# Turning r with VectorE from blocks instead of with TensorE, from the seventh chunk on

## The reference

```python
for t in range(S):
    cur = np.einsum('bhd,bhe->bhde', u[None] * kt, vt)
    y[:, :, t] = np.einsum('bhd,bhde->bhe', rt, state + cur)
    state = wt[:, :, :, None] * state + np.einsum('bhd,bhe->bhde', kt, vt)
...
h = x @ w_in                       # (3072, 384) @ (384, 2048)
g = np.maximum(0.01 * h, h)
x2 = g @ w_out
...
expert_idx = np.argmax(logits, axis=1)      # of the normalised x2 and 8 embeddings
h = np.maximum(x2[mask] @ w1[e], 0.0)
out[mask] = gate_w[mask, None] * (h @ w2[e])
```

## Time and profile before

| what | before |
|---|---|
| median of 3 runs | 835.03 us (833.4 to 835.28) |
| the profiled execution | 834.27 us, its span 832.3 us |
| granted TensorE clock, of full speed | 0.999 |
| TensorE matmuls busy | 814.6 us (98%) |
| VectorE busy | 564.4 us (68%) |
| ScalarE busy | 438.8 us (53%) |
| GpSimd busy | 203.3 us (24%) |

### The profile page before, as it was taken

One profiled execution on the slowest core, in us unless ns is written; L12 is line 12 of the kernel. 1 busy time (PEld: TensorE's weight loads), 2 busy tenths in 40 slices (PEclk: granted clock), 3 DMA queues, 4 the chain that ended last, 5 costly groups with the idle time before them and its releaser, 6 DMA issues.

```text
span 832.3 us, 18049 instructions
## 1 busy us (share of the span) xinstructions
PE 814.6 (98%) x5633; PEld 763.7 (92%) x5633; DVE 564.4 (68%) x1315; ACT 438.8 (53%) x924; POOL 203.3 (24%) x286
## 2 busy tenths in 40 slices
PE   6999999999999999999999999999999999999997
PEld 6899999999999999999999999999889998898896
DVE  6879788879889878879888855635452512545463
ACT  6675564464464465465456435553552533565563
POOL 5611111122103013103113001303343323334433
PEclk9999999999999999999999999999999999999999
DMA  9975432155242141232210001414531513376392
GB/s 215 206 150 130 77 68 39 34 92 69 51 73 34 31 84 33 39 83 38 39 34 30 1 16 30 171 47 128 168 124 40 185 47 100 134 259 201 92 315 66
DMA packets 165307, 78.56 MB, mean 94 GB/s; under 512 B 135486, under 2 KB 153253, under 8 KB 165090
## 3 DMA queue, kind: packets, MB, share of 16 engines
q1 hardware_dynamic: 156402, 64.81, 32.3%
q0 software_dynamic: 4544, 10.85, 4.0%
q10 hardware_dynamic: 4272, 1.82, 0.9%
HBM read 112.90 MB, written 11.63 MB: 150 GB/s over the span
## 4 chain that ended last, share of the span: by engine, by line
PE 85%; SPq 7%; DVE 3%; issue 2%; ACT 1%; DMA 1%; POOL 0%; DVEq 0%; ACTq 0%; POOLq 0%
PE bank L1065 22%; PE bank L1044 21%; PE bank L1117 13%; PE bank L1153 13%; SPq L458 3%; PE bank L1134 3%; PE bank L970 2%; PE bank L937 2%; PE bank L998 2%; PE bank L993 2%; SPq L483 1%; PE bank L1099 1%; PE bank L978 1%; SPq L471 1%; SPq L490 1%
## 5 line engine op out<-in xcount | busy, mean ns | idle before, releaser
L1044 PE MATMUL bank<-xhl,WRh 128*128 128x384 f32 x768 | 219.0, 339 | 0.7 <-DVE WRl L1715 0.5
L1044 PEld LDWEIGHTS bank<-xhl,WRh 128*128 128x128 f32 x768 | 141.3, 188 | 1.2 <-issue 1.2
L1411 ACT COPY gw<-bank 128x384 f32<-128x384 f32 x128 | 61.6, 481 | 152.3 <-PE bank L1044 150.9
L1065 PE MATMUL bank<-WRh,gh 128*128 128x384 f32 x384 | 135.8, 354 | 0.0
L1044 PE MATMUL bank<-xhl,WRl 128*128 128x384 f32 x384 | 130.0, 339 | 0.0
L1065 PE MATMUL bank<-WRh,gl 128*128 128x384 f32 x384 | 129.8, 338 | 0.0
L1065 PE MATMUL bank<-WRl,gh 128*128 128x384 f32 x384 | 129.7, 338 | 0.0
L1734 DVE TENSOR_TENSOR gl<-gw,gh 128x384 fp32r<-128x384 f32 x128 | 72.2, 564 | 56.6 <-ACT gh L1417 52.7
L1417 ACT CAST gh<-gw 128x384 fp32r<-128x384 f32 x128 | 65.2, 510 | 76.7 <-DVE gw L1727 64.4
L1727 DVE SCALAR_TENSOR_TENSOR gw<-gw 128x384 f32<-128x384 f32 x128 | 75.7, 592 | 31.3 <-ACT gw L1411 30.9
L1902 DVE TENSOR_TENSOR hl<-bank,hh 128x512 fp32r<-128x512 f32 x56 | 36.1, 686 | 84.0 <-ACT hh L1452 83.7
(11 more groups left out here) (199 smaller groups left out, 1639.7 us busy)
## 6 DMA issues: line engine op xcount, KB each, us to landing
stage<-in_moe_w_dram SPq DMA_DIRECT2D x96, 768.0 KB
Kn<-in_k_dram SPq DMA_DIRECT2D x24, 192.0 KB, 3.4
Vn<-in_v_dram SPq DMA_DIRECT2D x24, 192.0 KB, 3.2
x_moe<-x2s SPq DMA_DIRECT2D x24, 192.0 KB, 2.0
Rn<-in_r_dram SPq DMA_DIRECT2D x21, 192.0 KB, 2.8
wraw<-in_moe_w_out_dram SPq DMA_DIRECT2D x4, 768.0 KB, 7.4
eraw<-in_moe_w_dram SPq DMA_DIRECT2D x4, 768.0 KB, 8.9
Wn<-in_w_dram SPq DMA_DIRECT2D x152, 16.0 KB, 1.8
```

The source lines that it names most:

```text
L1044: mm = pe.matmul(bank[F_BANK[n % 2]][:, 0:GN], win(t_)[:, f // 4, k_, cols], xhl[G % 2][:, a, k_, :], start=(k_ == 0 and n_ == 0), stop=(k ...
L1065: mm = pe.matmul(bank[O_BANK[i]][:, 0:DM], a[:, z, cols], wout(t_)[:, f, :], start=(f == 0 and n_ == 0), stop=(f == FT - 1 and n_ == 2))
L1411: act.copy(gw[:, n % 2, :], bank[F_BANK[n % 2]][:, 0:GN]).then_inc(s_g0, 1)
```

## The change

From chunk 6 on (`R_BLOCKED = 2 * GT`), r is loaded twice: in its natural form as before, which GpSimd's `products` still need, and in blocks as w is, by 16 DMAs of `load_blocks`, into one of two further places of `Rn` (slot 3, a new one, and slot 2, freed for it). GpSimd clears the padding of these two (`s_pad`). VectorE's new `turn_r` turns the blocks in one instruction, from SBUF right into the bank from which `Rh` is made, at the head of `decay_rk`. TensorE turns only k, into the first of the three banks (`k_bank`) instead of the third. The waits that guarded r's and k's banks (`s_sx`, `s_yhi`, `s_ylo`) stand in front of the scores now. The natural r has two slots from chunk 6 on, so `next_load` waits for a later product. To make room, v has two slots instead of three; v of chunk m + 2 is asked for where v of chunk m + 3 was, and the first v loads move on SP: v of chunk 2 from the very start to where v of chunk 3 was, and so on.

```diff
+        R_BLOCKED = 2 * GT
+        def r_slot(m):
+            return m % NSLOT if m < R_BLOCKED else m % 2
+        def r_blocks(m):
+            return NSLOT - m % 2
+        def k_bank(m):
+            return banks(m)[0 if m >= R_BLOCKED else 2]
...
             def next_load(m):
 
                 sp.wait_ge(s_kT, m - NSLOT + 1)
-                sp.wait_ge(s_rk, m - NSLOT + 1)
+                sp.wait_ge(s_rk, m - NSLOT + 1 if m < R_BLOCKED else m - 1)
...
+            def next_r(m):
+
+                if m < R_BLOCKED + 2:
+                    sp.wait_ge(s_pad, m - R_BLOCKED + 1)
+                else:
+                    sp.wait_ge(s_rT, m - 1)
+                load_blocks(sp, m, r, Rn, r_blocks(m), s_rblk[m % 2])
...
             def next_v(m):
 
-                sp.wait_ge(s_ym, m - NSLOT + 1)
-                sp.wait_ge(s_sm, states(m - NSLOT + 1))
+                sp.wait_ge(s_ym, m - 1)
+                sp.wait_ge(s_sm, states(m - 1))
                 load_v(m)
...
             load_weights(0)
             next_load(GT)
-            next_v(GT)
+            next_v(GT - 1)
             load_weights(1)
...
             next_load(GT + 1)
+            next_v(GT)
             load_weights(2)
             next_v(GT + 1)
             load_weights(3)
             next_load(GT + 2)
-            next_v(GT + 2)
             next_w(GT + 2)
...
+                for m in at(turn_at, n - 2):
+                    if R_BLOCKED <= m + 2 < NC:
+                        next_r(m + 2)
...
                 if m > 2:
                     pe.wait_ge(s_mk, last + 1)
+                if 2 < m < R_BLOCKED:
                     pe.wait_ge(s_sx, states(last + 1))
-                turn_one(m, Rn, banks(m)[1], s_rT)
+                if m < R_BLOCKED:
+                    turn_one(m, Rn, banks(m)[1], s_rT)
...
-                turn_one(m, Kn, banks(m)[2], s_kT)
+                turn_one(m, Kn, k_bank(m), s_kT)
 
             def scores(m):
                 a_, b_, c_ = banks(m)
                 pe.wait_ge(s_rh, m + 1)
                 pe.wait_ge(s_kt, m + 1)
+                if m >= R_BLOCKED:
+                    pe.wait_ge(s_sx, states(m))
+                    pe.wait_ge(s_yhi, m)
+                    pe.wait_ge(s_ylo, m)
...
-                if f == 5 and G > 1 and (first or G == NG - 1):
+                if f == 5 and G > 1:
                     pe.wait_ge(s_slot, routes(first, G) - 1)
...
+            def turn_r(m):
+
+                dve.wait_ge(s_rblk[m % 2], 16 * 4 * HP * ((m - R_BLOCKED) // 2 + 1))
+                dve.wait_ge(s_ym, m - 1)
+                dve.transpose(bank[banks(m)[1]][:],
+                              Rn[:, r_blocks(m)].rearrange("p h d -> p (h d)")).then_inc(s_rT, 1)
...
             def decay_rk(m):
 
                 a_, b_, c_ = banks(m)
+                if m >= R_BLOCKED:
+                    turn_r(m)
                 dve.wait_ge(s_rT, m + 1)
```

More of the change, by code:

```diff
@@ L175, in build @@
         att = ExitStack()
-        Rn = sb("Rn", [P, NSLOT, H, HEAD_PAD], c=att)
+        Rn = sb("Rn", [P, NSLOT + 1, H, HEAD_PAD], c=att)
         Kn = sb("Kn", [P, NSLOT, H, HEAD_PAD], c=att)
         Wn = sb("Wn", [P, NSLOT, H, HEAD_PAD], c=att)
-        Vn = sb("Vn", [P, NSLOT, H, HEAD_PAD], c=att)
+        Vn = sb("Vn", [P, 2, H, HEAD_PAD], c=att)
         Fi = sb("Fi", [P, 2, HP, P + 1], c=att)
@@ L193, in build @@
         s_nat = [sem(f"s_nat{i}") for i in range(NSLOT)]
-        s_vin = [sem(f"s_vin{i}") for i in range(NSLOT)]
+        s_vin = [sem(f"s_vin{i}") for i in range(2)]
+        s_rblk = [sem(f"s_rblk{i}") for i in range(2)]
+        s_pad = sem("s_pad")
         s_wT = sem("s_wT")
@@ L454, in load_one, with load_blocks @@
         def load_one(eng, m, n_):
-            s_, (b, c) = m % NSLOT if n_ else w_slot(m), divmod(m, NCH)
+            s_, (b, c) = (w_slot(m), r_slot(m), m % NSLOT)[n_], divmod(m, NCH)
             dst, src = nat[n_]
             eng.dma_start(dst[:, s_, :, 0:D], src[b, :, c * P:(c + 1) * P, :].rearrange("h p d -> p h d")
-                          ).then_inc(s_nat[s_] if n_ else s_natw[s_], 16)
-        def load_blocks(eng, m):
-            s_, (b, c) = w_slot(m), divmod(m, NCH)
+                          ).then_inc(s_nat[m % NSLOT] if n_ else s_natw[s_], 16)
+        def load_blocks(eng, m, from_, dst, s_, done_):
+            b, c = divmod(m, NCH)
             for h in range(HP):
@@ L481, in load_v @@
             def load_v(m):
-                s_, (b, c) = m % NSLOT, divmod(m, NCH)
+                s_, (b, c) = m % 2, divmod(m, NCH)
                 sp.dma_start(Vn[:, s_, :, 0:D], v[b, :, c * P:(c + 1) * P, :].rearrange("h p d -> p h d")
@@ L512, in next_load @@
                     load_one(sp, m, 0)
+                elif m >= R_BLOCKED and m < R_BLOCKED + 2:
+                    sp.wait_ge(s_rT, m - 2)
                 load_one(sp, m, 1)
@@ L613, in mlp @@
                                 fill(m // GT)
-                            if m + NSLOT < NC:
-                                next_v(m + NSLOT)
+                            if m + 2 < NC:
+                                next_v(m + 2)
                         for m in blocks(block_at, n - 3):
@@ L807, in _ @@
             split_lo(1)
+            pool.memset(Rn[:, NSLOT].rearrange("p h d -> p (h d)"), 0.0).then_inc(s_pad, 1)
             def gather(j):
@@ L872, in mlp @@
                                 state(m)
+                        if n == turn_at[R_BLOCKED - 1] + 2:
+                            pool.wait_ge(s_rT, R_BLOCKED)
+                            pool.memset(Rn[:, NSLOT - 1].rearrange("p h d -> p (h d)"), 0.0).then_inc(s_pad, 1)
                     if f == 4 and 2 <= G < NG:
@@ L982, in sums @@
                 a_, b_, c_ = banks(m)
-                s_, z = m % NSLOT, m % 2
+                s_, z = m % 2, m % 2
                 pe.wait_ge(s_mk, m + 1)
-                pe.wait_ge(s_vin[s_], 16 * (m // NSLOT + 1))
+                pe.wait_ge(s_vin[s_], 16 * (m // 2 + 1))
                 if more(m) and m != 2:
```

18 lines of the change are left out of this document (9 added, 9 removed).

## The result

The changed kernel took 838.04 us (median of 8 runs, 835.67 to 839.76), the kernel before 834.02 us beside it on the same chip (8 runs, 833.4 to 835.28). The ratio is 1.0045, 95% interval [1.003, 1.0059]: 3.7 us slower by the ratio (4.0 by the medians), where 830.7 was forecast, with a range of 824.5 to 835.3.

The account below looks back on a forecast made before the run. The prediction took TensorE to bound the kernel, busy 814.6 of 832.3 us. Transposes -8.2, waits -2.4, chunk 7 +0.8 and feature 16 +6.2 gave -3.6, from 834.27 to 830.7 us, range 824.5 to 835.3.

Parts of the forecast that it names:

- TensorE's saving: TensorE, chunks 6 to 23: 72 transposes fewer save 8.6 us, three state sum waits gone save 2.4.
- VectorE's transpose: VectorE, ahead of `Rh` in each chunk from 6 on: one more transpose, 0.75 us, bounds 0.60 and 1.35.
- waits of the scores for `Kt` and `Rh`: TensorE's scores: chunk 7 waits 0.8 us for `Kt`; the cover suffices in the other chunks.
- What SP gains: SP's queue before the fill of group 1: added r loads make feature 16 start at 103.0, not 96.74, +6.2 us.
- the v load: SP ahead of chunk 5's w blocks: one v load fewer, -4.8 us, bounds -2.4 and -7.3.
- two r loads: SP ahead of the fill of group 1: two r block loads at 8.0 us each, +16.0, bounds 7.6 and 9.0 each.
- k and the loads between: SP ahead of the fill of group 1: k of chunk 8 issued faster than its 1.86 us, -0.6 us.
- The next group has SP back in time: Fill of group 2: TensorE comes some 5 us later than before, and SP about then.
- w of chunk 6: Ahead of feature 16: whatever is gained there is swallowed by the wait for the fill; no size given for this load.
- rival C: Feature 16: a fill landing from 106.5 us on, delay 9.8, eats the whole gain; 835 to 840 us; chance 0.12.
- B: Fill of group 1: SP catches up, landing at 99.0 us, total 826.8, or 824 without any wait; chance 0.24.
- D: VectorE sets the pace, each chunk adding 0.75 us where TensorE gives 0.44; 832 to 836 us; chance 0.14.

Follow-up runs that it names:

- e1: The changed kernel with the r block loads of chunks 6 and 7 left out, so its output is not the reference's; 825.48 us.
- e4: The kernel before with only v in two slots and its loads moved as in the change; 833.93 us.
- e5: The changed kernel with 72 idle transposes on TensorE ahead of its wait for the fill of group 1; 837.44 us.
- e11: The changed kernel with 72 idle transposes ahead of the group 1 fill wait and the 1.1 MB copy at step 100 instead of 36; 835.77 us.
- e9: The changed kernel with only the 1.1 MB copy moved, to step 100 instead of 36; 838.31 us.
- e2: The changed kernel with r of chunk 6 loaded behind w of chunk 6 and r of chunk 7 behind the fill of group 1; 835.49 us.
- e6: The changed kernel with r of chunk 6 behind w of chunk 6 and every group's third r load behind the fill; 834.11 us.
- e7: The changed kernel with the first two r block loads, chunks 6 and 7, issued by GpSimd instead of SP; 828.95 us.
- e10: e6 with the 1.1 MB copy issued at step 100 instead of 36; 828.27 us.

## Why the prediction was wrong, point by point

**TensorE's saving: right.** 72 instructions fewer. Behind step 17 the table shows 9.6 us of gain (+11.9 to +2.3); the terms gave 8.2 + 2.4 - 0.8 = 9.8. e1, without the wait, gives 9.0 in the medians.

**VectorE's transpose: right.** From SBUF into a bank it took 719 ns, about what the w transposes take (704 ns); I had 0.75. No transpose waited for its r blocks. In the order of line, duration ns min/median/max, first and last start:

```profile
L1673 DVE STREAM_TRANSPOSE bank<-Rn x18: 717/719/722, 100.5 to 475.8; 128x512 f32<-128x512 f32 x18
```

The waits of the scores for `Kt` and `Rh` are 1.3 and 0.9 us in three places; `Kt` had 1.0 before. So about 1.2 in place of 0.8; the 0.9 is at chunk 7, as forecast, but for `Rh`.

**The step that failed: "What SP gains", the start of feature 16.** Forecast 103.0, measured 106.79. By its terms, up to the end of k of chunk 8, where I had 88.74 + 10.6 = 99.34 and the row gives 102.87:

- the v load: forecast -4.8, measured -0.9 (w of chunk 5 ends at 58.44 instead of 59.34). This is most of the error, and it lies below even my bound of -2.4, as do the 0.9 to 2.2 us of the other kernels without this load. I took half of the w issues to stand in the full stretch, at their clean price; e4 shows that the w load grows by 4.85 of v's 6.26 us.
- two r loads: forecast 16.0, measured 9.25 + 7.92 and gaps, 17.4. (The prediction's 0.47 us per issue is that of a free queue; in the rows of 44 to 91 us it is 0.53 to 0.56.)
- k and the loads between: forecast -0.6, measured -2.4 (k and r of chunk 8 -1.3, the rest -1.1).

Sum +14.1 instead of +10.6. From there to feature 16 it is 3.9 instead of 3.65.

**A term that was missing: the clock.** The wait was forecast, but not that TensorE's clock would be at 1.2 GHz behind it; the sum has it at nothing, without a reason. It cost 1.8 us, tested by e5 and e11. Together: -3.6 + 3.8 (feature 16) + 1.8 (clock) + 0.2 (behind step 17) = +2.2, and the table ends at +2.3. With the error in feature 16's start alone the sum would be +0.2, no change; it takes both to make the kernel slower.

**What this account leaves open.** It is an account of one profiled execution of each kernel. These two lie 2.5 us apart, the medians 4.0. In e9, whose profiled execution is at its median, the clock cost 2.6 us and the table ends at +3.6. What the slower executions of the changed kernel lost beyond 2.5 us was not traced.

**"The next group has SP back in time": true, for a reason that makes it worth little.** It held because TensorE was late. e2 and e6 took most of the wait at step 16 away and got it back at 32 and 48. The forecast did not look at the copy at step 36, which the kernel before has too.

**w of chunk 6.** I let every loss ahead of feature 16 be swallowed by the wait for the fill, and so it is: the mask's 3.1 us put step 15 at +2.3, and the fill would not have come sooner without them. Where the wait for the fill is short, such a loss would count; that was not tested.

**The rivals.** What happened is nearest to rival C: place, sign and condition (a landing from 106.5 on; loads of 8.6 us, a v credit near its bound) are as written, and its 835 to 840 holds 838.04. That it holds it is in part luck: by C's own price, the delay of feature 16 less 9.8, the measured delay of 10.05 would cost 0.25 us, and the clock, which C leaves out, made the rest of the +2.3. I gave it 0.12, since I excluded a v credit near zero. That bound was argued from the w rows alone, and no row excluded that a full queue passes nearly all of its wait on. Rivals B and D did not occur; e1, where no fill is waited for, took 825.48, within B's 824 to 826.8.

## What to carry to other kernels

The time of a DMA issue in a full queue belongs mostly to the queue, not to the load in the row: taking the load out moved most of its time to the next one here (4.85 of 6.26 us), so credit little for it. Before adding issues to a queue, lay its timeline beside the points at which something behind it is needed, for every group and not for the first alone, and suppose that the first wait is mended; here the same change gives +3.7 us when it starts in the busy stretch, and -7.3 us when it starts six chunks later. And a wait of TensorE of some 2.5 us or more can have a second price, paid behind it in the clock: 1.4 to 2.6 us where the table of steps shows one.

## What the runs showed of the hardware that I had not expected

A load of 16 block issues takes 7.5 us at best and 12.8 to 16.8 us when the queue is full (12.82 and 16.80, both in e7); in the changed kernel's first such stretch the share of the DMA engines was 0.62, at 126 GB/s:

```profile
45.00:58.40 13.40, 12.96 (x88) 12.12 (x87) 10.92 (x23) 8.20 (x18) 2.95 (x3) 1.00 0.62 126
```

So the engines had room in the mean over all 16; what held the issues back the rows do not show. A copy of 1.1 MB is issued in 0.54 us, but the 16 small issues behind it then take 15.06 us instead of 8.36. After 8 us of idle TensorE was at half clock for some 4 us of work; in e5 it was so for 3.4 us behind a wait of 2.45 us, in e10 behind one of 3.2. GpSimd needs 8.7 to 9.0 us for the same 16 issues for which SP needs 7.5 to 9.5 outside the full stretches, and its product starts only when they are through.
